# Token groups of 2, 3, 3, 2, 2 tiles with products beside the scan from round 4 on, and unused identity products in rounds 0 to 3

## The reference

```python
for t in range(S):                                   # attention, state: (B,H,D,D)
    cur = einsum('bhd,bhe->bhde', u[None] * kt, vt)
    y[:, :, t] = einsum('bhd,bhde->bhe', rt, state + cur)
    state = wt[..., None] * state + einsum('bhd,bhe->bhde', kt, vt)
x = y as (B, S, 384)
xn = (x - mean) / sqrt(var + 1e-6) * g_ln            # over the last axis
x = x + maximum(xn @ w_ch1, 0) @ w_ch2
h = maximum(x @ w_in, 0); u, v = h[..., :512], h[..., 512:]
v_n = (v - mean(v)) / sqrt(var(v) + 1e-6)
v_s = einsum('ts,bsd->btd', w_spatial, v_n) + b_spatial[None, :, None]
out = (u * v_s) @ w_out
```

## Time and profile before

| | us |
|---|---|
| median of 3 runs | 429.52 (428.25 to 430.52) |
| the profiled execution's own time | 431.96 |
| its span, first to last instruction | 430.2 |
| PE busy | 403.0 |
| VectorE, ScalarE, GpSimd busy | 224.4, 147.6, 126.4 |

### The profile page before, as it was taken

How to read it: one execution, slowest core, us unless ns; L and a number is a source line. 1 busy time by engine, 2 the same in 40 slices (tenths; PEclk the granted TensorE clock), 3 DMA queues, 4 the chain that set the end, 5 groups by cost and what they waited for, 6 DMA issues and landing times.

```text
span 430.2 us, 12370 instructions
## 1 busy us (share of the span) xinstructions
PE 403.0 (94%) x5260; PEld 374.6 (87%) x5260; DVE 224.4 (52%) x492; ACT 147.6 (34%) x328; POOL 126.4 (29%) x149
## 2 busy tenths in 40 slices
PE   3687879999999999999999899999999999999997
PEld 2676668999999999999999799999988988989897
DVE  3889877666767666657543344133246934312120
ACT  3254544353432323232324422322327722211111
POOL 4656765636452323323220421001015400000000
PEclk9996885899999999999999999999999999999999
DMA  5658541412201020110000200000061100010102
GB/s 165 167 156 247 169 148 49 140 33 66 83 11 53 21 68 3 40 57 2 3 2 3 74 2 0 0 2 2 0 221 35 40 0 0 9 47 21 37 20 91
DMA packets 26555, 24.60 MB, mean 57 GB/s; under 512 B 1666, under 2 KB 23426, under 8 KB 26500
## 3 DMA queue, kind: packets, MB, share of 16 engines
q1 hardware_dynamic: 26500, 23.80, 18.3%
HBM read 21.44 MB, written 2.36 MB: 55 GB/s over the span
## 4 chain that ended last, share of the span: by engine, by line
PE 88%; DVE 5%; issue 3%; POOL 1%; ACT 1%; DMA 1%; SPq 0%; DVEq 0%; POOLq 0%; ACTq 0%
PE odd_bank L1259 11%; PE odd_bank L1261 9%; PE odd_bank L1260 9%; PE low_bank L1178 7%; PE low_bank L1259 6%; PE low_bank L1261 6%; PE low_bank L1260 6%; PE high_bank L1259 4%; PE high_bank L1260 4%; PE high_bank L1261 4%; PE bank L1226 3%; PE bank L1261 3%; PE bank L1260 3%; PE bank L1259 3%; PE bank L1222 2%
## 5 line engine op out<-in xcount | busy, mean ns | idle before, releaser
L611 POOL TENSOR_TENSOR kin<-kin,wtot 128x256 f32<-128x256 f32 x60 | 47.9, 803 | 65.8 <-PE low_bank L1178 59.8
L1178 PEld LDWEIGHTS low_bank<-rin,kin 64*64 64x64 f32 x1728 | 31.3, 144 | 17.7 <-DVE rin L876 7.1
L1178 PE MATMUL low_bank<-rin,kin 64*64 64x32 f32 x1728 | 35.7, 229 | 11.5 <-DMA rin<-in_rT 5.0
L876 DVE TENSOR_TENSOR rin<-rin,wtot 128x256 f32<-128x256 f32 x60 | 36.3, 609 | 14.3 <-PE low_bank L1178 12.2
L1006 DVE SCALAR_TENSOR_TENSOR h10l<-odd_bank,h10h 128x384 fp32r<-128x384 f32 x24 | 13.4, 557 | 44.7 <-ACT h10h L750 44.7
L628 POOL TENSOR_TENSOR vrstd<-vmv,half 128x1 f32<-128x1 f32 x12 | 7.7, 642 | 70.9 <-DVE vmv L1091 70.9
L609 POOL TENSOR_TENSOR kin<-kin,win 128x256 f32<-128x256 f32 x12 | 12.7, 1059 | 49.3 <-PE low_bank L1178 45.7
L918 DVE COPY_PREDICATED near<-msk,low_bank 128x256 f32<-128x256 int32 x54 | 27.0, 552 | 0.0
L1259 PE MATMUL odd_bank<-xnT0h,ffw 128*128 128x384 f32 x66 | 25.0, 379 | 0.0
L750 ACT ACTIVATE h11h<-odd_bank 128x384 fp32r<-128x384 f32 x16 | 7.9, 492 | 47.7 <-PE odd_bank L1261 47.7
L1260 PE MATMUL odd_bank<-xnT0l,ffw 128*128 128x384 f32 x66 | 22.7, 344 | 0.0
(11 more groups left out here) (252 smaller groups left out, 1158.0 us busy)
## 6 DMA issues: line engine op xcount, KB each, us to landing
kin<-in_kT SPq DMA_DIRECT2D x12, 256.0 KB, 3.2
rin<-in_rT SPq DMA_DIRECT2D x12, 256.0 KB, 4.5
win<-in_wT SPq DMA_DIRECT2D x12, 256.0 KB, 3.9
early_stage<-in_w SPq DMA_DIRECT2D x8, 384.0 KB, 4.0
vin<-in_v SPq DMA_DIRECT2D x12, 192.0 KB, 3.0
out<-ob SPq DMA_DIRECT2D x12, 192.0 KB, 1.9
stage<-in_w SPq DMA_DIRECT2D x4, 384.0 KB, 4.3
stage<-in_w_in SPq DMA_DIRECT2D x4, 384.0 KB, 3.3
```

Of the source, the lines that this page charges most:

```text
L611: last = gp.tensor_tensor(k, k, wr[:, :, :, None].to_broadcast([P, NPR, m, c]), ALU.mult)
L876: last = ve.tensor_tensor(r, r, wl[:, :, :, None].to_broadcast([P, NPR, m, c]), ALU.mult)
L1178: mm = te.matmul(dst[s0:s0 + Q, NPR * e + a, :], kin[i % 4][lo:hi, a, s0:s0 + Q], r[:, :, 1, :], start=True, stop=True)
```

## The change

The groups get the sizes 2, 3, 3, 2, 2 (`SIZE`, `FIRST`), so there are 60 F1 steps and 60 F2 steps, and the width of F1, its relu and U follows the group. `ALONE` becomes 3: F1 begins in round 4 (step 16), 36 F1 steps lie beside the scan and 24 after it, and tile 4's low levels have one PSUM bank. The weight pieces of w1 and w2 alternate, and `LO_SLOTS` has them earlier. Tiles 10 and 11 are transposed after the scan, and the last group's x2 transposes both go to F1's banks. `keep_going` issues three products of the identity with itself, into unused columns of y's bank, in steps 1 and 2 of rounds 0 to 3. The spatial products and the output keep groups of three.

```diff
-ALONE = 4
+ALONE = 3
+N_KEEP = 3
+    SIZE = [2, 3, 3, 2, 2]
+    NFG = len(SIZE)
+    FIRST = [sum(SIZE[:g]) for g in range(NFG + 1)]
-        FF_PIECES = [(w1, w1s, a) for a in W1_PIECES[:5]] + [(w2, w2s, W2_PIECES[0]), (w1, w1s, W1_PIECES[5])] + \
-                    [(w2, w2s, a) for a in W2_PIECES[1:]]
+        FF_PIECES = [(w1, w1s, a) for a in W1_PIECES[:KC]]
+        for a, b in zip(W2_PIECES, W1_PIECES[KC:]):
+            FF_PIECES += [(w2, w2s, a), (w1, w1s, b)]
+        FF_PIECES += [(w2, w2s, a) for a in W2_PIECES[KC:]]
-        LO_SLOTS = [(0, 0), (4, 5), (7, 9), (11, 13), (15, 16), (17, 18), (19, 20), (21, 22), (23, 24),
-                    (25, 26), (27, 28), (29, 30)]
+        LO_SLOTS = [(0, 0), (4, 5), (6, 7)] + [(9 + 2 * n, 10 + 2 * n) for n in range(N_FF - 3)]
+        X2T_AT = {0: 2, 1: 9, 2: 14, 3: 19}
+        V_AT = {0: 7, 1: 12, 2: 17, 3: 21}
+        U_AT = {0: 8, 1: 13, 2: 18}
         def ff_steps():
-            for n in range(N_BESIDE, NG * NF + 1):
+            for n in range(N_BESIDE, NFG * NF + 1):
+                m = n - N_BESIDE
...
-                if m == 1:
-                    yield "XT", NG - 1, TG - 1
+                if m in (0, 2):
+                    yield "XT", NFG - 1, m // 2
+                for g in range(NFG - 1):
+                    if 0 <= m - X2T_AT[g] < SIZE[g]:
+                        yield "X2T", g, m - X2T_AT[g]
...
-                sc.activation(h1[n % 2][0][:, :], f1_bank(n)[:, 0:GT], ACT.Relu).then_inc(h1_hi_ready, 1)
+                t = SIZE[n // NF] * P
+                sc.activation(h1[n % 2][0][:, 0:t], f1_bank(n)[:, 0:t], ACT.Relu).then_inc(h1_hi_ready, 1)
...
-                    split_vn(2 * a)
-                    split_vn(2 * a + 1)
+                    for c in range(CH // 2):
+                        split_vn(CH // 2 * a + c)
...
+                t = SIZE[g] * P
...
-                    mm = split_product(f1_bank(n)[:, 0:GT], w1s[0][:, w], w1s[1][:, w], xh[:, k, :], xl[:, k, :],
+                    mm = split_product(f1_bank(n)[:, 0:t], w1s[0][:, w], w1s[1][:, w], xh[:, k, 0:t], xl[:, k, 0:t],
...
-                for tt in range(TG):
+                for tt in range(SIZE[g]):
...
+            def keep_going(s):
+                if s >= 2:
+                    te.wait_ge(x_ready, s - 1)
+                else:
+                    te.wait_ge(consts_loaded, 48)
+                for _ in range(N_KEEP):
+                    te.matmul(b_y[:, D:BANK], idt[:, :], idt[:, :], start=True, stop=True)
...
                 n = f1_of(k)
+                if n is None and j in (1, 2):
+                    keep_going(s)
```

More of the change, by code:

```diff
@@ L59, in rwkv_moe_kernel @@
     GT = TG * P
+    SIZE = [2, 3, 3, 2, 2]
+    NFG = len(SIZE)
+    FIRST = [sum(SIZE[:g]) for g in range(NFG + 1)]
+    assert FIRST[NFG] == NT and max(SIZE) == TG
     W1C, W2C, WIC = KC * F1, NF * D, KC * DFF
@@ L171, in b_tr @@
         def b_tr(step, g, a):
-            return b_f1[a] if (step, g) == ("X2T", NG - 1) and a < 2 else b_turn
+            return b_f1[a] if (step, g) == ("X2T", NFG - 1) else b_turn
         w1s = [ffw[:, e * W1C:(e + 1) * W1C] for e in range(2)]
@@ L427, in weight_parts, with group_of @@
                         yield n, part
+        def group_of(i):
+            g = max(g for g in range(NFG) if FIRST[g] <= i)
+            return g, i - FIRST[g]
+        X2T_AT = {0: 2, 1: 9, 2: 14, 3: 19}
+        V_AT = {0: 7, 1: 12, 2: 17, 3: 21}
+        U_AT = {0: 8, 1: 13, 2: 18}
         def ff_steps():
-            for n in range(N_BESIDE, NG * NF + 1):
-                if n < NG * NF:
+            for n in range(N_BESIDE, NFG * NF + 1):
+                m = n - N_BESIDE
+                if n < NFG * NF:
                     yield "F1", n // NF, n % NF
@@ L448, in ff_steps @@
             for d in range(ND):
[L449 to L453, removed]
+                yield "U", NFG - 2, d
+                if d < SIZE[NFG - 1]:
+                    yield "X2T", NFG - 1, d
+            for tt in range(SIZE[NFG - 1]):
+                yield "V", NFG - 1, tt
             for d in range(ND):
-                yield "U", NG - 1, d
+                yield "U", NFG - 1, d
         STEPS = list(ff_steps())
-        TR_STEPS = [("XT", i // TG, i % TG) for i in range(NT - 1)] + [s for s in STEPS if s[0] in ("XT", "X2T")]
+        TR_STEPS = [("XT",) + group_of(i) for i in range(NT - 2)] + [s for s in STEPS if s[0] in ("XT", "X2T")]
         def hi_parts_of(t):
@@ L773, in _ @@
             take_x(NT - 1)
[L775 removed]
+            tr, vu = NT - 2, 0
             for step, g, a in STEPS:
@@ L1026, in add_f2 @@
                 dve.wait_ge(f2_done, NF * (g + 1))
-                for tt in range(TG):
-                    i = TG * g + tt
+                for tt in range(SIZE[g]):
+                    i = FIRST[g] + tt
                     ve.tensor_tensor(x[:, i, :], b_acc[tt][:, 0:D], x[:, i, :], ALU.add).then_inc(x2_ready, 1)
@@ L1091, in _ @@
                     ve.tensor_scalar(vmv[:, i, 1:2], vmv[:, i, 1:2], EPS, None, ALU.add).then_inc(v_var_ready, 1)
-                    if g == NG - 1:
-                        split_vn(2 * a)
-                        split_vn(2 * a + 1)
+                    if g == NFG - 1:
+                        for c in range(CH // 2):
+                            split_vn(CH // 2 * a + c)
                     dve.wait_ge(v_rstd_ready, i + 1)
@@ L1100, in _ @@
                     vu += 1
-                if step == "X2" and g == NG - 1:
+                if step == "X2" and g == NFG - 1:
                     weight_lo(N_LATE)
-                elif step == "U" and g == NG - 2:
+                elif step == "U" and g == NFG - 2:
                     weight_lo(N_LATE + 2 + a)
-                elif step == "U" and g == NG - 1 and a < 2:
+                elif step == "U" and g == NFG - 1 and a < 2:
                     weight_lo(N_ALL - 2 + a)
@@ L1249, in turn @@
                 if t and b_tr(step, g, a) is b_turn:
-                    te.wait_ge(turned_lo_ready, t if (step, g) != ("X2T", NG - 1) else t - 2)
+                    te.wait_ge(turned_lo_ready, t)
                 for k in range(KC):
@@ L1321, in _ @@
                     gain(s - 2)
-                if j == 2 and s >= 2:
-                    turn(s - 2, "XT", (s - 2) // TG, (s - 2) % TG)
+                if j == 2 and 2 <= s < NT:
+                    turn(s - 2, "XT", *group_of(s - 2))
                 if j == 3 and s >= 1 and carries(s - 1):
                     turn_k(s - 1)
-            tr, vu = NT - 1, 0
+            tr, vu = NT - 2, 0
             for step, g, a in STEPS:
```

73 lines of the change are left out of this document (36 added, 37 removed).

## The result

The changed kernel takes 436.60 us (median of 4 runs, 433.30 to 437.86) against 430.02 (4 runs, 428.25 to 430.73) beside it: 1.0147 of the time before, 95% interval 1.0097 to 1.0196. Run again on another chip it took 435.06, 1.0093 of before (1.0071 to 1.0115). Forecast was 424.9, with a range of 419.5 to 431.5. The change is slower, and the forecast had it faster.

What follows compares the result with a forecast made beforehand. PE was taken to bound 355 us, the scan running nearly alone for about 75. Early part +0.5, rounds 4 to 6 -7.3, round 7 -0.5, after the scan +2.7 gave -4.6 us: 424.9 from median 429.52, range 419.5 to 431.5.

Steps and rivals of the forecast that it cites:

- `gain(0)` late by ScalarE's order: Round 2's start: ScalarE meets chunk 3's load ahead of `take_kt`, so `gain(0)` starts near 35.3 instead of 31.48: +3.8 us.
- The narrow products: F1 on two-tile groups: 256-column products take 0.120 us each, nine 1.08 us against 1.56 for three tiles.
- Weight loads don't hold them at 0.173: Rival, chance 0.03: weight loads pace narrow F1 and U products at 0.173 us, +23 us, total 448.
- -2.4 for round 3: Round 3: identity products keep PE's clock full, shortening attend, transpose, own terms and last level by 2.4 us.
- +0.8: Rounds 0 to 3: GpSimd's 13 half-chunks instead of 9 push round 3's levels and inverse deviation: +0.8 us.
- The signs that were to show the forecast wrong: `gain(0)` not late, PE idle over 3 us in rounds 4 to 6, or 256-column products not near 0.12.
- rounds 4 to 6, -7.3: Rounds 4 to 6: two-tile feed-forward beside the scan from round 4 takes 49.4 us against 56.7: -7.3 us.
- my 1.5: Rounds 4 to 6: allowance of 1.5 us for waits on VectorE and single low-level banks.
- rounds 4 to 6 are not PE's: Rival, chance 0.16: VectorE and GpSimd hold the low levels, 17.8 us a round, gain 4.5 smaller, total 429.4.
- early stretch doesn't warm: Rival, chance 0.12: rounds 2 and 3 stay at slow clock, early part +7.8 us, total 432.
- after the scan, +2.7: After the scan: F1, U, a stall with ScalarE's load, and late VectorE, less a shorter wait: +2.7 us.
- The identity products, +0.7: Rounds 0 to 3: calls cost 0.65 us at full clock, 1.3 at slow; +0.7 us in all, one call exposed.

Runs made afterwards that it cites:

- e1: Changed kernel, but ScalarE rounds both halves of weight chunk 2 in step 5 and of chunk 3 in step 8: 432.01 us, 1.0029 of the kernel before.
- second execution: The unaltered changed kernel, profiled again on another chip (span 433.1 us); its median there 435.06 us, 1.0093 of the kernel before.
- first execution: Profiled execution of the unaltered changed kernel from its first measurement, whose median was 436.60 us, 1.0147 of the kernel before.
- e4: Kernel before, with only the identity products added in steps 1 and 2 of rounds 0 to 3: 430.15 us, 0.9990.
- e3: Changed kernel without the identity products: 433.42 us, 1.0066 of the kernel before.
- e12: e7 with feed-forward beside the scan from round 5 instead of 4, half-chunks in the kernel before's steps, after-scan steps renumbered: 433.11 us, 1.0064.
- e5: Changed kernel with the first group's x2 transposes, X2T(0,0), one step later: 433.21 us, 1.0060 of the kernel before.
- e8: e7 with VectorE writing the turned xn's low part ahead of the own-term select in step 3: 425.94 us, 0.9903; again 426.89.
- e6: e2 without the identity products: 431.21 us, 1.0019 of the kernel before.
- e2: Changed kernel with GpSimd's weight half-chunks, and by them ScalarE's, at later steps: 431.11 us, 1.0019 of the kernel before.
- e10: e7 without the identity products: 428.36 us, 0.9954 of the kernel before.
- e7: Changed kernel with both the later half-chunks of e2 and the later x2 transposes of e5: 428.10 us, 0.9939 of the kernel before.
- e9: e7 with no GpSimd half-chunk in steps 12 to 15, which are round 3: 426.89 us, 0.9940 of the kernel before.

## Why the prediction was wrong

**Right, and shown.** `gain(0)` late by ScalarE's order: forecast +3.8, measured +3.9 (35.36 for 31.48), undone by `e1`. In the second execution, ScalarE:

```profile
34.31 0.51 ACT L710 CAST ffw<-early_stage 128x384 fp32r<-128x384 f32 x1 [5.13 <-DMA early_stage<-in_w]
34.73 0.58 ACT L751 COPY kt<-bank 128x512 f32<-128x512 f32 x1
```

The load landed as in the earlier trace rows. In the first execution it landed 1.5 us later (35.82), which is the larger part of the 2.1 by which that one is longer. The wait of 1.15 in the earlier trace rows went, and `gain(0)` to round 3 is 1.0 shorter. The narrow products, PE's timeline of the first execution:

```profile
83.26 0.28 PE L1279 MATMUL odd_bank<-xnT0l,ffw 128*128 128x256 f32 x1
...
84.10 0.28 PE L1280 MATMUL odd_bank<-xnT0h,ffw 128*128 128x256 f32 x1
```

Seven steps from the one to the other in 0.84 us: 0.120 each, as forecast. Weight loads don't hold them at 0.173, and round 6, with four steps of two tiles, takes 16.5 us against 20.31, nearly the 1.0 a step of the sum.

**The step that failed: "-2.4 for round 3".** The sum took PE's clock as round 3's bound. The clock came as forecast (0.96 to 1.00) and the round grew by 1.2 us. The saving needed VectorE to be ready, and VectorE already had 10.7 of 13.1 us in that round and was done with its low part only 0.9 us before PE started `turn_k`, which waits for it. Forecast -2.4, measured +1.2: 3.6 of the 7.5 us. `e4` splits them. There, with the full clock and the half-chunks of the kernel before, the round is 0.2 us shorter and not 2.4, since PE waits 1.72 for VectorE: 2.2 us. The other 1.4 (14.24 for 12.84) come in the changed kernel with its earlier half-chunks. I had counted them (+0.8) on GpSimd's own path alone; what they did was to lengthen VectorE's instructions beside them (12.3 us for the 26, where they took 11.35 in `e4`), and the low part came 1.4 us later. That PE's clock isn't the bound is seen from the other side in `e3`: without the identity products the clock in round 3 is 0.76, the wait at `turn_k` 0.63 us, and the round takes 14.26 us all the same. The split rests on one execution of each kernel; `e12` repeats the 12.84 and `e5` the 14.2.

The signs that were to show the forecast wrong did not cover this term: `gain(0)` was late, PE idled 1.5 us and not 3 in rounds 4 to 6, the products took 0.12. The one sign that spoke was the start of round 4, forecast near 58 and measured at 61.5 and 63.1.

**Mis-sized: rounds 4 to 6, -7.3.** They take 53.0 us in the first execution and 52.4 in the second, for the forecast 49.4. Part is the clock that falls after the wait at `turn_k`, in the first execution:

```profile
62.00:66.00 4.00, 3.92 (x73) 3.55 (x74) 1.29 (x4) 1.38 (x3) 1.64 (x2) 0.50 0.28 82
```

PE is 98% busy there, at half speed. `e3`, with the same half-chunks and a full clock in all three rounds, takes 51.3; `e8`, warm too, 51.2. So 1.1 to 1.7 us are the clock. Of the 1.9 that are left, 0.6 are idle time above my 1.5, and 1.3 are PE's own work. More than half of that is an error of the sum: its base, round 6 with 20.31 us, is a round without `turn_k`, since with tile 6 the second sequence begins and tile 5 hands no state on. Rounds 8 to 10 of the kernel before have it and take 20.72 each:

```profile
133.64:154.36 20.72, 20.72 (x384) 19.49 (x384) 14.52 (x34) 7.39 (x18) 6.38 (x8) 1.00 0.13 38
```

Rounds 4 and 5 have it too, which makes 0.8 us. The rival "rounds 4 to 6 are not PE's" gave 17.8 us a round, and 17.7 is the mean; that it comes so near is luck, as PE idles 0.6, 0.7 and 0.2 us in the three rounds, no more than the sum allowed. The rival "early stretch doesn't warm" came nearest to the total (432 for 436.6 and 435.1), but for the wrong reason: round 3 was warm, and slow.

**Mis-sized: after the scan, +2.7.** Measured +4.1. The 1.4 us are the half clock after the stall: `e3`, with the stall and the full clock, has +2.5. `e4` has the fall with the old steps, so this part differs between executions and can't be laid to the change. The single terms of this sum were not measured one by one.

**The identity products, +0.7.** One call of three, at half and at full clock, in the changed kernel:

```profile
38.89 1.65 PE L1329 MATMUL bank<-idt 128*128 128x128 f32 x6
...
51.82 0.94 PE L1329 MATMUL bank<-idt 128*128 128x128 f32 x6
```

I had 1.3 and 0.65. By the four passes of the Trainium skill (FP8 and Floating Point Precision, section TensorE Precision Notes) a call is an estimate of 0.64 us. The rows have 0.94 with its modelled end, and 0.77 and 0.87 from a call's start to the next instruction's in `e4`; the measurement decides. That the calls neither cost nor bring anything that the medians can tell (`e4`, `e6` against `e2`, `e10` against `e7`) has two reasons in the traces: a faster PE in round 3 waits for VectorE, and in the changed kernel the clock then falls in round 4, where without them it doesn't.

**Readings.** PE's busy digits in the earlier trace rows are 9 from the seventh slice on, with an 8 once, counted from one; the prediction has them from slice 8. Its slices of the slow clock, 3 to 7, are counted from zero.

**Open.** PE's pauses of 0.9 to 1.9 us without a releaser, in attend of rounds 2 and 3; why chunk 3 landed at 34.3 in one execution and 35.8 in another; why the clock fell after some of the stalls of 2 us and not after others.

## What to carry to other kernels

A faster clock is worth what the next engine leaves of it: before a saving is booked to one engine, add up how late each of its partners would be, in the round in question, with the work that the change gives them. Work moved to an engine off the path can lengthen the instructions of another that is on it. And where an engine takes its orders in sequence, a load that lands late must not stand ahead of the copy on which the next stage waits; that one was forecast to 0.1 us from a timeline alone.

## What the runs showed of the hardware

Some VectorE instructions that start beside one of GpSimd's last until about 0.2 us after GpSimd's is done: `sdec` 1.15 us instead of 0.35, and after the scan the normalisation of 384 columns:

```profile
240.18 2.13 DVE L975 TENSOR_SCALAR xn<-x,mv,rstd 128x384 f32<-128x384 f32 x1
```

```profile
240.25 1.85 POOL L637 TENSOR_TENSOR inw<-stage,inw 128x768 fp32r<-128x768 f32 x1 [0.95 <-ACT inw L710]
```

2.13 us, where the shortest of its twelve takes 0.46, ending with GpSimd's (242.31 and 242.10). It isn't so each time. The `sdec` of `e9` starts 0.08 us ahead of an instruction of GpSimd's and keeps its 0.35; the normalisation above starts 0.07 ahead, and doesn't. And before, a `select` out of PSUM (51.58) takes its usual 0.43 us in the midst of one of GpSimd's (51.33 to 52.13). The Trainium skill (GPSIMD Engine Reference, section Specifications) says that GpSimd shares its SBUF interfaces with VectorE, and that they contend when VectorE has two SBUF inputs or runs in a perf mode with two ports. For `sdec`, with two inputs in SBUF, and for the `select` the trace agrees; in which mode the normalisation ran no run shows.

PE's clock fell to 1.2 GHz after single stalls of 2.07 and 2.22 us in a stretch that was full before and after, and after the wait of 1.76 us at the end of round 3. It stayed at 2.4 GHz after stalls of 1.97, 2.15 and 2.38 us in the same place of other kernels (but fell after one of 1.97 in `e4`), and after the wait of 1.41 in `e8`.
